# The factor weights of an attention and routing kernel, loaded from ScalarE's queue instead of SyncE's

## The reference

```python
# 1: linear attention, B=H=4, S=1088, head_dim 32, S1 and S2 are 8 x 32
phi(x) = outer(S1 @ x, S2 @ x)            # 64 features for a token and head
kv, z = phi(k).T @ v, sum(phi(k))
x = (phi(q) @ kv) / (phi(q) @ z + 1e-6)   # -> 4352 tokens x 128
# 2: greedy routing by x @ w_gate to 8 experts of capacity 544, then
x[mask_e] = relu(x[mask_e] @ w1[e]) @ w2[e]
# 3: soft mixture of experts with 32 slots over the same tokens
```

## Time and profile before

| | us |
|---|---|
| median of 3 runs | 342.2 |
| lowest and highest | 341.83 and 343.26 |
| the profiled execution, its own time | 343.21 |
| the span of that execution's trace | 341.5 |

### The profile page before, as it was taken

One profiled execution on the slowest core, in us unless ns is written; L12 is line 12 of the kernel. 1 busy time (PEld: TensorE's weight loads), 2 busy tenths in 40 slices (PEclk: granted clock), 3 DMA queues, 4 the chain that ended last, 5 costly groups with the idle time before them and its releaser, 6 DMA issues.

```text
span 341.5 us, 6748 instructions
## 1 busy us (share of the span) xinstructions
PE 295.6 (87%) x2577; PEld 226.4 (66%) x2577; DVE 207.6 (61%) x860; ACT 94.0 (28%) x200; POOL 87.6 (26%) x105
## 2 busy tenths in 40 slices
PE   6999999953334479999999999999999998999992
PEld 3789989942223257777777777777677786755471
DVE  4615287997789858787788787787864002202162
ACT  1312033420000022242251242232332534313345
POOL 5000010000000600631641551452366363302300
PEclk9999999995555559999999999999999998999998
DMA  6999702222003130122131130140142210000207
GB/s 236 404 411 422 301 2 61 63 61 77 3 0 125 32 126 2 33 53 83 33 95 41 34 132 3 33 133 7 29 131 97 65 29 12 6 2 2 65 10 261
DMA packets 15039, 31.72 MB, mean 93 GB/s; under 512 B 2848, under 2 KB 8864, under 8 KB 13984
## 3 DMA queue, kind: packets, MB, share of 16 engines
q1 hardware_dynamic: 11584, 27.46, 22.4%
q0 software_dynamic: 2560, 2.79, 3.2%
q10 hardware_dynamic: 864, 1.05, 0.9%
HBM read 26.28 MB, written 5.01 MB: 92 GB/s over the span
## 4 chain that ended last, share of the span: by engine, by line
PE 71%; DVE 15%; POOL 4%; issue 4%; DMA 3%; ACT 3%; ACTq 0%; SPq 0%; DVEq 0%; POOLq 0%
PE psum L524 18%; PE psum L532 17%; PE psum L419 5%; PE psum L432 5%; PE psum L618 4%; PE psum L403 3%; POOL kq_sb L371 3%; DVE feats L1129 2%; PE psum L551 2%; PE psum L697 2%; PE psum L564 2%; DVE feats L944 1%; PE psum L628 1%; DMA kq_sb<-x_by_token,tokens 1%; DVE x L1042 1%
## 5 line engine op out<-in xcount | busy, mean ns | idle before, releaser
L371 POOL DMA_INDIRECT kq_sb<-x_by_token,tokens x40 | 42.7, 1067 | 114.5 <-DVE tokens L1108 100.7
L834 ACT ACTIVATE v_flat<-psum 128x544 f32<-128x544 f32 x64 | 39.9, 624 | 101.9 <-PE psum L524 101.9
L381 POOL DMA_INDIRECT slot_logits_by_token<-kq_sb,tokens x40 | 39.0, 976 | 63.6 <-ACT kq_sb L863 53.8
L1129 DVE TENSOR_TENSOR feats<-digit_pad,steps 128x640 bf16<-128x640 int16 (+1 forms) x86 | 43.5, 539 | 0.3
L524 PE MATMUL psum<-kq_sb 128*128 128x272 f32 x128 | 39.7, 425 | 0.9 <-ACT kq_sb L827 0.9
L618 PE MATMUL psum<-mask_pad,feats 128*128 128x32 bf16 (+1 forms) x490 | 21.5, 179 | 20.9 <-DVE feats L1129 18.0
L532 PE MATMUL psum<-v_flat,kq_sb 128*128 128x272 f32 x128 | 39.2, 414 | 0.0
L524 PE MATMUL psum<-kq_sb,v_flat 128*128 128x272 f32 x128 | 38.6, 423 | 0.0
L532 PE MATMUL psum<-v_flat 128*128 128x272 f32 x128 | 37.9, 411 | 0.4 <-ACT v_flat L834 0.4
L618 PEld LDWEIGHTS psum<-mask_pad,feats 128*128 128x128 bf16 x490 | 18.7, 99 | 27.7 <-DVE feats L1129 12.8
L944 DVE TENSOR_TENSOR feats<-ab 128x2048 f32<-128x2048 f32 (+1 forms) x10 | 19.6, 1963 | 12.6 <-PE psum L432 7.6
(11 more groups left out here) (233 smaller groups left out, 462.9 us busy)
## 6 DMA issues: line engine op xcount, KB each, us to landing
u_sb<-u SPq DMA_DIRECT2D x8, 1024.0 KB, 19.3
kq_sb<-wts SPq DMA_DIRECT2D x8, 512.0 KB, 4.5
v_flat<-wts SPq DMA_DIRECT2D x8, 512.0 KB, 4.7
kq_sb<-kT SPq DMA_DIRECT2D x4, 512.0 KB, 5.9
v_flat<-v SPq DMA_DIRECT2D x4, 512.0 KB, 6.7
kq_sb<-qT SPq DMA_DIRECT2D x4, 512.0 KB, 8.9
x_by_token<-x SPq DMA_DIRECT2D x4, 512.0 KB, 3.2
out<-x SPq DMA_DIRECT2D x4, 256.0 KB, 2.3
```

What stands on the lines that cost most here:

```text
L371: pool.indirect_dma_start(out=xg[0:rows, b, :], out_offset=None, in_=x_dram, in_offset=bass.IndirectOffsetOnAxis(ap=tokens[0:rows, which, ...
L381: pool.indirect_dma_start(out=l2_dram, out_offset=bass.IndirectOffsetOnAxis(ap=tokens[0:rows, which, b:b + 1], axis=0), in_=l2_now[0:rows, ...
L834: act.activation(hT[:, f % 2].rearrange("p (b t) -> p b t", b=2), psum[:, 2 + 2 * (f % 2):4 + 2 * (f % 2), 0:HALF], ACT.Relu)\
L1129: dve.tensor_tensor(above[:, a * P:z * P].rearrange("p (g j c) -> p g j c", j=shape[2], c=side), digit_pad[:, a * side:z * side].rearrange ...
```

## The change

The fill of `siT` goes from the head of GpSimd's stream to behind its constants. `wab` alone now signals `zeroed`; `wgz` has a semaphore of its own, for which SyncE waits only ahead of line 282's DMAs. The four DMAs of `wab` go from SyncE's stream to the head of ScalarE's, behind a wait for `zeroed`. SyncE issues the values of group 0 right behind the keys of group 0. In the diff "names" is the list of semaphores.

```diff
-                 "share_ready h2t_ready h2t_copied so8_ready zeroed consts vone_ready ab_ready "
+                 "share_ready h2t_ready h2t_copied so8_ready zeroed wgz_zeroed consts vone_ready ab_ready "
@@ @block.sync
             sp.dma_start(kT_sb[:, 0:AB_GROUP * P], kT[:, 0:AB_GROUP * P]).then_inc(loaded_k[0], 16)
-            sp.wait_ge(S["zeroed"], 2)
-            for h in range(HEADS):
-                sp.dma_start(wab[h * HD:(h + 1) * HD, 2 * h * R:(2 * h + 2) * R], s12T).then_inc(S["loaded_w"], 16)
             for g, tiles in enumerate(KGROUPS):
...
+            sp.wait_ge(S["wgz_zeroed"], 1)
             for h in range(HEADS):
                 hp, j = h // 2, h % 2
                 sp.dma_start(wgz[j * HV:j * HV + HD, hp, j * EXPERTS:(j + 1) * EXPERTS],
@@ @block.gpsimd
-            pool.memset(siT[:], 0.0).then_inc(S["sit_zeroed"], 1)
             pool.memset(wab[:], 0.0).then_inc(S["zeroed"], 1)
-            pool.memset(wgz[:], 0.0).then_inc(S["zeroed"], 1)
+            pool.memset(wgz[:], 0.0).then_inc(S["wgz_zeroed"], 1)
...
+            pool.memset(siT[:], 0.0).then_inc(S["sit_zeroed"], 1)
             pool.wait_ge(S["kv_ready"], BATCH)
@@ @block.scalar
+            act.wait_ge(S["zeroed"], 1)
+            for h in range(HEADS):
+                act.dma_start(wab[h * HD:(h + 1) * HD, 2 * h * R:(2 * h + 2) * R], s12T).then_inc(S["loaded_w"], 16)
             act.wait_ge(S["warm_ready"], 1)
             act.copy(act_table[:], ones_b[:, 0:1])
```

## The result

| | before | changed |
|---|---|---|
| median, us (14 runs each) | 341.45 | 344.41 |
| lowest to highest, us | 340.27 to 343.26 | 342.68 to 344.98 |
| the profiled execution, us | 343.21 | 343.5 |
| its span, us | 341.5 | 341.8 |
| wait for `wab`, us | 0.9 | 2.6 |

The ratio is 1.0073, with a 95% interval of 1.0057 to 1.0089: 1.9 to 3.0 us slower. The profiled executions differ by 0.3 us only. That is the first thing to explain, and it has to be explained from the stretches, not from the spans.

What follows compares the result with a forecast made beforehand. TensorE's chain was taken as bound by the landing of `wab`'s last block: +2.4 us for the landing, zero for fills, ScalarE's stream and clock, so 342.2 + 2.4 = 344.6 us, range 340.9 to 346.0.

Steps and rivals of the forecast that it cites:

- What bounds the kernel: TensorE's start: the last `wab` block's landing shifts everything after it; earlier gains at most 0.9 us, later costs its whole delay.
- Fills, `wgz`, the siT fill: GpSimd and SyncE: `wab`'s fill done 0.25 us earlier; `siT`'s 0.31 us falls in idle time; nothing queues behind `wgz`'s wait.
- ScalarE's stream: ScalarE's head: four issues at 1.0, 1.45, 1.9 and 2.36 us; table load and small copy behind them, hidden by 7.66 us idling.
- The rival with the table load first: ScalarE's head: block issues start only at 2.10 us, keys 2 and values 2 go ahead, +5.0 us, 347.2; chance 0.13.
- The landing: `wab`'s last block: lands behind three of SyncE's loads, at 8.6 instead of 6.15 us, +2.4; +1.1 if one load less.
- the strict order of issue: DMA queues: each block waits for every load issued before it, at 1.3 us per 512 KB load.
- the rival of 341.3: DMA engines: blocks slip through between SyncE's loads, the last landing at 4.9 to 5.3 us, 0.9 gained; chance 0.27.
- The sum: Whole kernel: span 341.5 + 2.4 = 343.9 us, 345.6 for a like execution, 344.6 as the median.
- this case's own range: Whole kernel, blocks landing behind the loads: 343.3 to 345.9 us around 344.6; this case's chance 0.50.
- The median: Whole kernel: median 1.0 us below the profiled execution's time, so 342.2 + 2.4 = 344.6 us.
- The clock term: TensorE's sixteen constant products: a later start shifts them whole, zero taken; ends 1.3 us back or 1.1 added.

Runs made afterwards that it cites:

- e5: The kernel before with 4 instead of 8 constant products ahead of the wait for `wab`: 342.12 us, ratio 1.0008.
- e6: The changed kernel with 4 instead of 8 constant products ahead of the wait for `wab`: 343.48 us, ratio 1.0060.
- e3: The changed kernel's fills and wait for `wgz`, with the four `wab` blocks back in SyncE's stream: 341.50 us, ratio 1.0010.
- e2: The changed kernel with ScalarE's four block issues moved behind its small copy: 345.2 us, ratio 1.0108 to the kernel before.
- e1: The changed kernel with SyncE waiting, after keys 0, until ScalarE has issued its four blocks: 341.87 us, ratio 1.0018 to the kernel before.
- e11: The changed kernel run again, nothing altered: 343.88 us, ratio 1.0064 to the kernel before.
- e4: The changed kernel with 14 instead of 8 constant products ahead of the wait for `wab`: 340.36 us, ratio 0.9970 to the kernel before.
- e8: The kernel before with e3's fills and queue, keys 1 issued ahead of values 0, and 10 constant products: 337.27 us, ratio 0.9869.

## Why the prediction was right

**What bounds the kernel.** Right. TensorE has one wait for a DMA up to 60 us in both traces, and in e5 and e6 1.5 us at the first factors is 1.65 us at 112 us and 1.71 at 293.

**Fills, `wgz`, the siT fill.** Right, at nothing that e3 can tell (at most 0.25%). `siT` took 0.30 us of idle time at 4.74.

**ScalarE's stream.** The issues start at 0.99, 1.41, 1.88 and 2.35, as worked out, and the table load follows at 2.99. The rival with the table load first is out; and e2 shows that its price was wrong too, since there the issues started while the table load was running.

**The landing.** Right in its core: the blocks land later because of the loads that SyncE issues beside them. e1 takes those away and most of the loss is gone. The size is off. I took 8.6 us for the last block, behind values 1, with 7.3 as the other end; it was 7.8 and 7.9 in the profiles. The step that failed is the strict order of issue, "a DMA waits for the one that was issued before it" and "two queues don't share the engines packet by packet": block 4 landed 1.1 us ahead of values 1, a load issued before it, the last block of e2 passed a load as well, and packets of both queues stand in the same slices of 0.2 us from 4.8 to 7.6 us. The stores of the earlier trace rows were 256 KB each, with no small DMA among them. The Trainium skill (DMA: Bandwidth & Descriptors, Queues, rings and completion order) has the engines take turns between queues, a packet of descriptors at a time, and I had set that against the scatter of the earlier trace rows. The mixed slices and the passing agree with turns; but several blocks in one turn behind the first keys, from which the rival of 341.3 drew its gain, did not happen beside a stream: the blocks landed at 4.7, 5.9, 6.9 and 7.8. (In e1, without one, 153 of the 192 packets did pass within 0.8 us.) The strict order gives 8.6, and a landing with keys 0 about 5; what puts the last block at 7.8 was not settled.

**The sum.** The predicted cost was 2.4 us, from a landing 2.4 us later. (The upper end of this case's own range should have read 342.2 + 3.5 = 345.7, not 345.9.) The landing is 1.65 us later in the two profiles (1.5 in e5 and e6), and the ratios say 2.5 us (1.9 to 3.0) and, in e11, 2.2 (1.4 to 3.0). So the sum came out right with one term too large by 0.8 us and something of about that size missing. That the total fits is luck in this part. The clock was the candidate, with an early rise that helps the kernel before more. The pair with 4 products gives 1.4 to 1.8 us instead of 2.5, as it should be then. But the executions of the kernel before that had a mean clock of 0.903 to 0.905, the mark of an early rise, took 341.7 us on average, no less than the others, and the intervals of e6, e11 and the main result overlap. The clock's return at 126.7 or 129.2 us, worth 1.0 us, is another candidate, seen in one pair of traces only and absent from e5 and e6 (26.05 and 26.14 us from the first to the sixth gather). This part stays open.

**The median.** I predicted 342.2 + 2.4 = 344.6, and 344.41 was measured. The base of that sum was high by 0.75 us, since 14 runs put the kernel before at 341.45; this made up, by luck, for a difference that was 0.56 us larger than forecast. A forecast of the difference alone would have been 2.4 against 2.96 by the medians and 2.5 by the ratio.

**The clock term.** I took zero and -1.3 to +1.1 as ends. For the sixteen products it was -1.3 in the profile pair (5.79 to 4.50 us) and -0.8 in e11 (4.95). Nothing in the prediction foresaw what the clock did later in the same pair, +1.0 us at 126 to 129 and -1.5 around 289. Together these hid almost all of the loss from anyone who compares the two spans.

## What to carry to other kernels

A small load that gates the whole kernel belongs in front of the bulk loads, not beside them: on a queue of its own it was issued 0.3 us earlier here and still landed 1.65 us later, among the 512 KB loads that another engine had pushed meanwhile. If it must be moved to another queue, hold the bulk loads back until it is issued (e1, within 0.2% of the kernel before), and read the landing, not the issue. And where the first products run at the lower clock, look at what raises the clock ahead of them first: six more constant products were worth more here (3.5 to 4 us in e4) than what the queue lost. And don't take the difference of two traces' spans for the worth of a change: take marks along the way, and see where the granted clock differs.

## What the runs showed that I had not expected

- More constant products ahead of the factors (14 in e4, 10 in e8) let the clock rise ahead of them, and the factors ran at the upper level even behind waits of 1.4 and 0.4 us: both groups took 3.79 us. In the kernel before, with 8, TensorE then worked without a gap for 11 us at the lower level, factors among it, and they took 7.09.
- An early rise can be lost again, as the two groups of e3 show (2.15 and 3.27 us). In e2 the granted clock reads full while TensorE waited and half while it worked. The 1.00 is weak evidence, since the column reads full from the start in each trace, also where the products run at the lower level; the 0.50 agrees with factors of 7.09 us (columns as above):

```profile
5.30:8.50 3.20, 0.00 (x0) 0.00 (x0) 0.51 (x6) 0.00 (x0) 0.00 (x0) 1.00 1.04 416
8.70:18.80 10.10, 10.10 (x40) 8.08 (x41) 5.17 (x11) 3.06 (x4) 0.00 (x0) 0.50 1.04 400
```

- About 3 us at half clock, somewhere between 245 and 292 us and with TensorE busy, stand in ten of the thirteen traces and cost 1.5 to 2.0 us each where the marks show it. What brings them was not looked into.
- ScalarE issued DMAs at 1.66 us while its table load ran from 0.82 to 2.10 (e2).
